# Moving two weight splits to GpSimd, dropping the pre-filled pad rows, and reordering the hand-over to the expert stage

## The chip, the core and the metric

The kernel runs on one core of a Trainium2 chip. The metric is the device time of one execution in microseconds (us). The engines are named as in the profile: PE is TensorE, DVE is VectorE, ACT is ScalarE, POOL is GpSimd, SP is SyncE, which here only issues DMAs. PEld is the weight load of TensorE, which overlaps with PE.

## The reference

Three stages run one after the other, all in fp32. The first is a linear attention with a decay for each head (batch 4, 8 heads, 768 positions, head size 64). The second is an MLP with a leaky ReLU whose slope is given for each feature (3072 tokens, 512 to 2048 to 512). The third is a mixture of 8 experts, in which each token goes to the one expert with the highest score.

```python
# attention, for each position t
state = gamma * state + outer(k[t], v[t]);  y[t] = scale * q[t] @ state
# MLP
h = x @ w_in;  g = maximum(h, 0) + alpha * minimum(h, 0);  x = g @ w_out
# experts
logits = normalise(x) @ normalise(expert_emb).T / tau
expert_idx = argmax(logits);  gate_w = softmax(logits)[expert_idx]
for e in range(8):
    mask = expert_idx == e
    out[mask] = gate_w[mask] * (maximum(x[mask] @ w1[e], 0) @ w2[e])
```

## The kernel before

**Products in parts.** A product in full precision is made of three matmuls of a high part (the value rounded to fp32r) and a low part (the value minus its high part): high by high, high by low, low by high. So each operand is split once. ACT makes the high part with a copy, and DVE or POOL makes the low part with a subtraction.

**Attention and MLP.** The 768 positions are 6 chunks of 128 (`NC = 6`), each with the 4 batches side by side, so that a chunk has 512 tokens. For each chunk come the attention (4 head pairs) and then the MLP, which this text calls an MLP pass. A pass has 16 blocks `f` of 128 hidden features. In block f, PE computes `hidden(f+1)` (12 matmuls, line 675) and `down(f)` (12 matmuls, line 684). DVE forms the leaky ReLU from the hidden product in lines 898 and 903, ACT makes its high part (line 1266) and POOL its low part (`g_lo`, line 1478; in blocks 0 and 15 DVE makes it, line 909). `down(f)` waits for the low part.

**The router in the next pass.** The scores of chunk c are computed during the MLP pass of chunk c + 1, on DVE, as products of 512 columns summed into one number (line 960): 4 in each of the blocks 1 to 7, 2 in the blocks 0 and 8, one in eight of them with an operand in PSUM. They follow the leaky ReLU of the same block in DVE's order. In blocks 9 to 12 DVE normalises, chooses the expert, and computes the table row of each token. POOL scatters the rows to their places in a table in DRAM (`scatter`, line 1496) with an indirect DMA. In the passes before the last one, POOL also scales queries and values for the next attention (lines 1461 and 1456) behind `g_lo` in blocks 3, 5, 6, 8 and 11.

**The table.** Each expert has a region of 3200 rows (`CAP`). Tokens are read from it in tiles of 128 rows, and the rest of an expert's last tile must hold pad rows. For this the kernel before writes 512 pad rows (`FILL`) at the start of each region, in the second chunk (line 506, 8 DMAs of 1028 KB), and once the counts are known 128 more behind the tokens of each expert (`pads`, line 380, 8 DMAs of 257 KB, each after a `value_load` of its address). So the tiles 2 and 3, which lie in the first 512 rows of the first expert, are loaded ahead of `pads` (`load_rows`, line 367), and tile 4 after it. The first expert, the one with most tokens, is chosen two chunks early (`choose_first`); its tiles 0 and 1 are loaded in the last MLP pass.

**The first expert's weights.** Four pieces `raw[0..3]` of 128x2048 are loaded and split in the last MLP pass: ACT makes the high parts in blocks 4, 5, 11 and 12 (`HI_AT`), and DVE the low parts in blocks 11 to 14 (`LO_VECTOR_AT`, `split_raw`, line 1026), counted in the semaphore `s_plV`.

**The expert stage.** For each tile t, PE computes `up(t, half)` twice (12 matmuls each, line 759), transposes the ReLU of it (`h_transpose(t)`, line 770), and computes `expert_down(t)` (24 matmuls, line 785). ACT and DVE each make one half of the ReLU (`relu_half`), and then the high (`h_hi_part`, line 1365) and the low part (`h_lo_part`, line 1130) of its transpose. `x_transpose(t)` (line 660) turns the token rows, and `x_hi_part` and `x_lo_part` split them. `y_part(t)` scales the result. The output bank is one, so `expert_down(t + 1)` waits for `y_part(t)`.

**The hand-over.** The order of each engine is written out by hand (lines 801 to 829 for PE, 1142 to 1203 for DVE, 1383 to 1402 for ACT, 515 to 541 for SP). PE does `up(0,0)`, transposes the rows of the last chunk and computes its logits with 32 matmuls of 8 columns (line 639), then `up(0,1)`, the rank and the counts (lines 646, 647 and 810), `up(1,0)`, `h_transpose(0)`, `up(1,1)`, and then the first down products. DVE turns the counts into the tile table: line 1160 writes the pad addresses (`s_pt`), and line 1195 the last entries (`s_tab`). Loads of token rows from tile 2 on wait for the table, and so does `up(2)`.

## Time and profile before

| | us |
|---|---|
| median of 3 executions | 992.1 |
| lowest, highest | 989.66, 993.94 |
| the profiled execution | 989.66 |
| its span, first to last instruction | 987.8 |
| PE busy in the span | 960.6 (97%) |
| DVE, ACT, POOL busy | 579.2, 256.5, 241.3 |
| share of PE in the chain that ended last | 88% |
| mean granted clock of TensorE, of full speed | 0.993 |

The profiled execution was also the fastest of the three. Its span leaves out 1.9 us around the instructions. An engine's busy time is the union of its instructions, so 97% says that PE has little idle time left, and not that its matmuls run at their peak. "Idle before" an instruction is told with its releaser, the instruction whose semaphore came last. A duration of POOL or DVE contains the time in which it was held back by the other one. The granted clock is 1.00 at 2.4 GHz and 0.50 at 1.2 GHz.

### The profile page before, as it was taken

How to read it: one execution, taken by the hardware profiler on the slowest of the kernel's cores; microseconds unless marked ns; L12 is line 12 of the kernel's file. 1: busy time of each engine (PE TensorE's matmuls, PEld its weight loads, DVE VectorE, ACT ScalarE, POOL GpSimd, SP SyncE). 2: the span in 40 equal slices, each digit the busy share in tenths (PEclk: the TensorE clock that was granted, in tenths of full speed). 3: DMA queues.
4: the chain of work that ended last, by engine and by line, in shares of the span. 5: the costliest groups of instructions: out<-in, count | busy, mean ns of one | idle time of the engine just before them, and what ended most of it. 6: DMA issues, size and time to landing. Idle time of an engine off the chain costs nothing.

```text
span 987.8 us, 16560 instructions
## 1 busy us (share of the span) xinstructions
PE 960.6 (97%) x5448; PEld 794.4 (80%) x5449; DVE 579.2 (59%) x1079; ACT 256.5 (26%) x405; POOL 241.3 (24%) x192
## 2 busy tenths in 40 slices
PE   7999999999999999999999999999999999999994
PEld 6788778888887888878887888877888888888883
DVE  4655579637973698459864878664332742524541
ACT  4222121112111211122111212332333533423541
POOL 3443114241433133413441224210000110000000
PEclk9999999999999999999999999999999999999998
DMA  7431393023001400140011203446331361423310
GB/s 283 157 139 55 116 370 114 1 86 129 0 0 73 140 0 0 43 149 1 1 44 54 107 35 134 130 136 249 128 128 43 150 262 43 175 75 121 125 44 31
DMA packets 27122, 100.48 MB, mean 102 GB/s; under 512 B 4383, under 2 KB 4767, under 8 KB 22448
## 3 DMA queue, kind: packets, MB, share of 16 engines
q1 hardware_dynamic: 19136, 80.64, 22.8%
q0 software_dynamic: 4336, 12.61, 3.3%
q10 hardware_dynamic: 3600, 6.58, 2.4%
q8 instruction: 29, 0.48, 0.2%
q14 instruction: 21, 0.17, 0.1%
HBM read 87.19 MB, written 24.20 MB: 113 GB/s over the span
## 4 chain that ended last, share of the span: by engine, by line
PE 88%; DVE 4%; DMA 2%; SPq 1%; ACT 1%; issue 1%; POOL 1%; ACTq 0%; DVEq 0%; POOLq 0%
PE bank L684 25%; PE bank L675 25%; PE bank L759 14%; PE bank L785 14%; PE bank L571 2%; PE bank L770 2%; PE bank L617 2%; PE bank L587 1%; PE bank L660 1%; PE bank L604 1%; DMA en_all<-en_rows 1%; DVE scratch L898 1%; DVE scratch L903 1%; DMA en_all<-in_qk 1%; DVE activations_split L909 1%
## 5 line engine op out<-in xcount | busy, mean ns | idle before, releaser
L684 PE MATMUL bank<-weights_split,activations_split 128*128 128x512 f32 x1152 | 278.7, 391 | 4.9 <-DVE activations_split L909 4.7
L675 PE MATMUL bank<-activations_split,weights_split 128*128 128x512 f32 x1152 | 277.5, 391 | 0.4 <-issue 0.4
L684 PEld LDWEIGHTS bank<-weights_split,activations_split 128*128 128x128 f32 x1152 | 215.2, 188 | 54.6 <-DVE activations_split L909 7.8
L675 PEld LDWEIGHTS bank<-activations_split,weights_split 128*128 128x128 f32 x1152 | 215.1, 188 | 45.8 <-issue 1.5
L1478 POOL TENSOR_TENSOR activations_split<-scratch,activations_split 128x512 fp32r<-128x512 f32 x84 | 118.0, 1405 | 332.5 <-ACT activations_split L1266 325.1
L1266 ACT CAST activations_split<-scratch 128x512 fp32r<-128x512 f32 x96 | 59.8, 622 | 418.1 <-DVE scratch L903 418.1
L785 PE MATMUL bank<-weights_split,activations_split 128*128 (+1 forms) x648 | 154.9, 394 | 3.0 <-DVE activations_split L1130 2.2
L759 PE MATMUL bank<-weights_split,activations_split 128*128 (+1 forms) x648 | 156.8, 398 | 0.5 <-DVE activations_split L1107 0.5
L785 PEld LDWEIGHTS bank<-weights_split,activations_split 128*128 128x128 f32 x648 | 119.6, 188 | 27.5 <-issue 3.6
L759 PEld LDWEIGHTS bank<-weights_split,activations_split 128*128 128x128 f32 x648 | 121.3, 191 | 24.8 <-issue 0.7
L960 DVE SCALAR_TENSOR_TENSOR attention<-rows,en_all 128x512 f32<-128x512 f32 x140 | 135.0, 1006 | 0.0
L898 DVE TENSOR_SCALAR scratch<-bank,alpha 128x512 f32<-128x512 f32 x96 | 71.8, 748 | 105.6 <-PE bank L675 101.6
L1532 POOL DMA_INDIRECT out<-scratch,y_token x27 | 29.1, 1079 | 297.9 <-ACT scratch L1375 297.9
L1130 DVE TENSOR_TENSOR activations_split<-bank,activations_split 128x512 fp32r<-128x512 f32 x54 | 34.8, 686 | 111.2 <-ACT activations_split L1365 111.1
L903 DVE SCALAR_TENSOR_TENSOR scratch<-bank,scratch 128x512 f32<-128x512 f32 x96 | 66.4, 692 | 3.3
L1121 DVE TENSOR_TENSOR weights_split<-attention,weights_split 128x2048 f32 (+1 forms) x21 | 47.6, 2288 | 15.5 <-ACT weights_split L1346 15.5
L1114 DVE TENSOR_SCALAR en_all<-bank 128x512 f32<-128x512 f32 x27 | 18.6, 690 | 50.2 <-PE bank L759 50.2
L863 DVE SCALAR_TENSOR_TENSOR attention<-bank,constants 128x512 f32<-128x512 f32 x44 | 28.4, 686 | 33.2 <-PE bank L571 33.2
L1375 ACT ACTIVATE scratch<-bank,rows 128x512 f32<-128x512 f32 x25 | 17.2, 687 | 93.8 <-PE bank L785 93.8
L1365 ACT CAST activations_split<-bank 128x512 fp32r<-128x512 f32 x54 | 29.0, 590 | 42.7 <-issue 29.6
L1346 ACT CAST weights_split<-attention 128x2048 f32 (+1 forms) x21 | 39.4, 1912 | 0.1
L1496 POOL DMA_INDIRECT expert_rows<-rows,slot_i x24 | 25.4, 1060 | 31.1 <-issue 28.3
(183 smaller groups left out, 678.4 us busy)
## 6 DMA issues: line engine op xcount, KB each, us to landing
attention<-in_w_exp SPq DMA_DIRECT2D x24, 1024.0 KB, 4.8
attention<-in_kv SPq DMA_DIRECT2D x43, 256.0 KB, 3.8
expert_rows<-in_pad_rows SPq DMA_DIRECT2D x8, 1028.0 KB, 18.3
en_all<-in_w_exp SPq DMA_DIRECT2D x8, 1024.0 KB, 7.1
rows<-in_w_mlp SPq DMA_DIRECT2D x14, 512.0 KB, 3.4
rows<-expert_rows ACTq DMA_DIRECT2D x25, 257.0 KB, 2.7
attention<-in_qk SPq DMA_DIRECT2D x12, 512.0 KB, 4.9
scratch<-in_qk SPq DMA_DIRECT2D x10, 512.0 KB, 3.7
```

Of the source, the lines that this page charges most:

```text
L675: last = mm(H_ps[f % 2][:, :], win(a, kc, f), x[:, kc, :], start=(k == 0), stop=(k == 3 * KC - 1))
L684: last = mm(bank[j][:, :], x[f % 2][:, j * P:(j + 1) * P], wout(a, f), start=(f == 0 and n == 0), stop=(f == FB - 1 and n == 2))
L759: last = mm(EH_ps[half][:, :], x[tt % 2][:, kc * P:(kc + 1) * P], W[:, bass.ds(slot * HALF + w1_at(kc, a) + half * 512, 512)], start=(k == ...
L785: last = mm(EY_ps[:, :], x[tt % 2][:, fc * P:(fc + 1) * P], W[:, bass.ds(slot * HALF + w2_at(fc, a), DM)], start=(k == 0), stop=(k == 3 * ...
L898: ve.tensor_scalar(neg, H_ps[f % 2][:, :], 0.0, alpha_sb[:, f:f + 1], ALU.min, ALU.mult)\
L903: ve.scalar_tensor_tensor(g_sb[f % 2], H_ps[f % 2][:, :], 0.0, neg, ALU.max, ALU.add)\
L960: ve.scalar_tensor_tensor(dot_out[n % 2], xrow[j][:, 0:DM], 1.0, EN[:, e * DM:(e + 1) * DM] if e < E - 1 else EN_ps, ALU.mult, ALU.mult, a ...
L1121: ve.tensor_tensor(W[:, bass.ds(at_ + CH, CH)], raw[m], W[:, bass.ds(at_, CH)].bitcast(f32), ALU.subtract).then_inc(s_lo[m // HC], 1)
L1130: ve.tensor_tensor(eh_lo[tt % 2][:, half * 512:(half + 1) * 512], HT_ps[half][:, :], eh_hi[tt % 2][:, half * 512:(half + 1) * 512].bitcast ...
L1266: se.copy(g_hi[f % 2], g_sb[f % 2]).then_inc(s_gh, 1)
L1346: se.copy(W[:, bass.ds((e % 2) * HALF + raw_at(m), CH)], raw[m]).then_inc(s_hi[m // HC], 1)
L1478: gp.tensor_tensor(g_lo[f % 2], g_sb[f % 2], g_hi[f % 2].bitcast(f32), ALU.subtract)\
```

## The change

- The 8 DMAs with 512 pad rows each are gone (`FILL`, `s_fill`, and the scatter's wait for it), and the pad array has 128 rows. `table_done` now also waits for `s_pads`; SP issues `pads` first, and then the rows of tiles 2, 3 and 4.
- The low parts of pieces 0 and 1 of the first expert are made on POOL in four halves of 128x1024, in blocks 5 to 8 of the last MLP pass, behind `g_lo`. DVE keeps pieces 2 and 3 in blocks 13 and 14.
- PE: `up(1,0)` comes ahead of the rank and the counts; `h_transpose(1)` comes behind `expert_down(0)` and no longer in the middle of it.
- DVE: `h_lo_part(0)` comes earlier in the table's chain, and `relu_half(1)` and the split of expert 1's piece 0 come behind its end, ahead of `h_lo_part(1)`.
- ACT: `y_part(0)` comes ahead of `h_hi_part(1)`, whose wait is now for `expert_down(0)`.

```diff
-    FILL = pad_rows.shape[0]
@@ table_done
         eng.wait_ge(s_tab, due(s_tab, 1))
+        eng.wait_ge(s_pads, due(s_pads, 16 * E))
@@
     HI_AT = {4: 0, 5: 1, 11: 2, 12: 3}
-    LO_VECTOR_AT = {11: 0, 12: 1, 13: 2, 14: 3}
+    LO_POOL_AT = {5: (0, 0), 6: (0, 1), 7: (1, 0), 8: (1, 1)}
+    LO_VECTOR_AT = {13: 2, 14: 3}
@@ sync
             chunk(1)
-            for e in range(E):
-                sp.dma_start(table[e * CAP:e * CAP + FILL, :], pad_rows[:, :]).then_inc(s_fill, 16)
             with sp.Fori(2, NC - 2) as c:
@@
                 sp.wait_ge(s_phi, due(s_phi, m + 1))
-                sp.wait_ge(s_plV, due(s_plV, m + 1))
+                if m < 2:
+                    sp.wait_ge(s_plP, due(s_plP, 2 * m + 2))
+                else:
+                    sp.wait_ge(s_plV, due(s_plV, m - 1))
                 load_raw(e, m)
-            table_done(sp)
-            load_rows(sp, 0, 2)
-            load_rows(sp, 0, 3)
             pads(sp)
             sp.wait_ge(s_pad0, due(s_pad0, 16))
-            sp.wait_ge(s_pads, due(s_pads, 16 * E))
-            load_rows(sp, 1, 0)
+            table_done(sp)
+            for t in range(2, 5):
+                load_rows(sp, t // 4, t % 4)
@@ tensor
             pe.wait_ge(s_phi, due(s_phi, 2))
-            pe.wait_ge(s_plV, due(s_plV, 2))
+            pe.wait_ge(s_plP, due(s_plP, 4))
             up(0, 0, 0, 0)
@@
             up(0, 0, 1, 0)
+            up(1, 1, 0, 0)
             router_rank(NC - 1)
             mm(CNT_ps, ones, seen[:, :, B], start=True, stop=True).then_inc(s_cnt, 1)
-            up(1, 1, 0, 0)
             h_transpose(0)
             up(1, 1, 1, 0)
             pe.wait_ge(s_phi, due(s_phi, NCH))
-            pe.wait_ge(s_plV, due(s_plV, NCH))
-            expert_down(0, 0, 0, between=lambda: h_transpose(1))
+            pe.wait_ge(s_plV, due(s_plV, 2))
+            expert_down(0, 0, 0)
+            h_transpose(1)
             expert_down(1, 1, 0, between=lambda: x_transpose(0, 2))
@@ vector
-            ve.scalar_tensor_tensor(tab[o, T_PADS:T_PADS + E], cnt[o, :], float(FILL), base[o, :], ALU.max, ALU.add).then_inc(s_pt, 1)
+            ve.tensor_tensor(tab[o, T_PADS:T_PADS + E], cnt[o, :], base[o, :], ALU.add).then_inc(s_pt, 1)
...
             link(ve.tensor_reduce(cnt_at[o, 0:1], eq_first[o, :], AX, ALU.add))
+            h_lo_part(0, 0)
...
             link(ve.tensor_copy(tab[o, T_EXP:T_EXP + TILES], eid[o, 1:TILES + 1]))
-            h_lo_part(0, 0)
...
             link(ve.tensor_scalar(tab[o, T_ROW:T_ROW + TILES], row_f[o, :], row_first[o, 0:1], float(PAD), ALU.add, ALU.min))
-            relu_half(1)
...
             ve.tensor_copy(tab[o, T_NEXT:T_NEXT + TILES], nx[o, :]).then_inc(s_tab, 1)
+            relu_half(1)
+            split_expert(1, (0,))
             h_lo_part(1, 1)
-            split_expert(1, (0,))
             x_lo_part(2, 2)
@@ scalar, h_hi_part and the order
-                    act.wait_ge(s_M2, due(s_M2, t - 1 if isinstance(t, int) and t == 1 else t))
+                    act.wait_ge(s_M2, due(s_M2, t))
...
             split_expert(1, (2, 3))
+            y_part(0, 0, 0)
             h_hi_part(1, 1)
-            y_part(0, 0, 0)
@@ gpsimd, mlp
+                    if is_last(c) and f in LO_POOL_AT:
+                        split_raw(*LO_POOL_AT[f])
@@
+            def split_raw(m, half):
+
+                pool.wait_ge(s_phi, due(s_phi, m + 1))
+                at_, n = raw_at(m) + half * CH // 2, CH // 2
+                gp.tensor_tensor(W[:, at_ + CH:at_ + CH + n], raw[m][:, half * n:(half + 1) * n],
+                                 W[:, at_:at_ + n].bitcast(f32), ALU.subtract).then_inc(s_plP, 1)
+
             def scatter(c, tiles=range(B)):
                 pool.wait_ge(s_rk, due(s_rk, c + 1))
-                pool.wait_ge(s_fill, due(s_fill, 16 * E))
@@ host
-    pad_rows = np.zeros((4 * P, DM + 2), np.float32)
+    pad_rows = np.zeros((P, DM + 2), np.float32)
```

## Rows read from the trace of the kernel before

**Rows 1.** Timeline, last MLP pass, blocks 5 and 6 (start us, length us, engine).

```profile
570.00 0.75 DVE L898 TENSOR_SCALAR scratch<-bank,alpha 128x512 f32<-128x512 f32 x1 [0.77 <-PE bank L675]
...
572.21 1.64 POOL L1478 TENSOR_TENSOR activations_split<-scratch,activations_split 128x512 fp32r<-128x512 f32 x1 [4.15 <-ACT activations_split L1266]
...
575.24 2.88 PE L684 MATMUL bank<-weights_split,activations_split 128*128 128x512 f32 x12
575.44 0.75 DVE L898 TENSOR_SCALAR scratch<-bank,alpha 128x512 f32<-128x512 f32 x1 [0.42 <-PE bank L675]
```

**Rows 2.** Timeline, the MLP pass before it, blocks 5 to 8.

```profile
466.59 0.75 DVE L898 TENSOR_SCALAR scratch<-bank,alpha 128x512 f32<-128x512 f32 x1 [0.21 <-PE bank L675]
...
472.35 0.74 DVE L898 TENSOR_SCALAR scratch<-bank,alpha 128x512 f32<-128x512 f32 x1
...
475.80 1.75 POOL L1461 TENSOR_TENSOR attention<-attention,constants 128x512 f32<-128x512 f32 x1
...
478.02 0.74 DVE L898 TENSOR_SCALAR scratch<-bank,alpha 128x512 f32<-128x512 f32 x1
...
485.14 1.30 POOL L1478 TENSOR_TENSOR activations_split<-scratch,activations_split 128x512 fp32r<-128x512 f32 x1 [3.30 <-ACT activations_split L1266]
...
486.39 1.05 POOL L1456 TENSOR_TENSOR attention<-attention,constants 128x512 f32<-128x512 f32 x1
```

**Rows 3.** All instructions of line 1510; duration in ns.

```profile
L1510 POOL TENSOR_TENSOR weights_split<-scratch,weights_split x1: 2360/2360/2360, 16.7 to 16.7; 128x1024 fp32r<-128x1024 f32 x1
```

**Rows 4.** Timeline, last MLP pass, blocks 11 to 14.

```profile
608.35 2.88 PE L684 MATMUL bank<-weights_split,activations_split 128*128 128x512 f32 x12
...
610.71 2.28 DVE L1026 TENSOR_TENSOR weights_split<-attention,weights_split 128x2048 fp32r<-128x2048 f32 x1
610.76 3.38 POOL L1478 TENSOR_TENSOR activations_split<-scratch,activations_split 128x512 fp32r<-128x512 f32 x1 [4.56 <-ACT activations_split L1266]
...
614.19 3.04 PE L684 MATMUL bank<-weights_split,activations_split 128*128 128x512 f32 x12 [0.24 <-POOL activations_split L1478]
...
625.47 2.88 PE L684 MATMUL bank<-weights_split,activations_split 128*128 128x512 f32 x12
```

**Rows 5.** Busy us of PE, PEld, DVE, ACT, POOL; granted clock, DMA share, GB/s.

```profile
640.00:646.00 6.00, 6.00 (x18) 4.84 (x17) 2.91 (x19) 1.09 (x2) 0.00 (x0) 0.50 0.00 0
```

**Rows 6.** Timeline of TensorE, from the last logits to the fourth up product.

```profile
640.13 5.47 PE L759 MATMUL bank<-weights_split,activations_split 128*128 128x512 f32 x12
...
652.83 2.89 PE L785 MATMUL bank<-weights_split,activations_split 128*128 128x512 f32 x12
...
660.18 2.99 PE L785 MATMUL bank<-weights_split,activations_split 128*128 128x512 f32 x12 [0.82 <-issue]
...
663.01 0.60 PE L660 MATMUL bank<-constants,rows 128*128 128x128 f32 x4
...
673.19 1.09 PE L770 MATMUL bank<-constants,en_all 128*128 128x128 f32 x8 [0.96 <-ACT en_all L1341]
...
674.78 5.72 PE L759 MATMUL bank<-weights_split,activations_split 128*128 x24 [0.49 <-DVE activations_split L1107]
```

**Rows 7.** Timeline of VectorE in that stretch.

```profile
647.28 0.15 DVE L1160 SCALAR_TENSOR_TENSOR tile_table<-cnt,constants 1x8 int32<-1x8 f32 x1
...
654.95 0.17 DVE L1195 CAST tile_table<-nx 1x31 int32<-1x31 f32 x1
```

**Rows 8.** Timeline of SyncE's DMA issues in that stretch.

```profile
655.92 1.42 SPq L367 DMA_DIRECT2D rows<-expert_rows  x2
658.12 10.16 SPq L380 DMA_DIRECT2D expert_rows<-in_pad_rows  x8
```

**Rows 9.** The chain that ended last, one piece (start us, length us, what).

```profile
667.75 3.71 DMA expert_rows<-in_pad_rows
```

**Rows 10.** DMA issues by line: count, size, median us to landing.

```profile
rows<-expert_rows SPq DMA_DIRECT2D x3, 257.0 KB, 2.6
```

**Rows 11.** Timeline of TensorE, second MLP pass, first down product.

```profile
134.68 3.01 PE L684 MATMUL bank<-weights_split,activations_split 128*128 128x512 f32 x12 [1.97 <-DVE activations_split L909]
```

More of the change, by code:

```diff
@@ L293, in build @@
     s_emb_ld, s_en_st, s_en_all, s_en_last = sem("emb_ld"), sem("en_st"), sem("en_all"), sem("en_last")
-    s_star, s_tail, s_fill = sem("star"), sem("tail"), sem("fill")
+    s_star, s_tail = sem("star"), sem("tail")
     s_lg = sem("lg")
@@ L311, in build @@
     s_raw = [sem(f"raw{i}") for i in range(4)]
-    s_phi, s_plV = sem("phi"), sem("plV")
+    s_phi, s_plV, s_plP = (sem(n) for n in ("phi", "plV", "plP"))
     s_hi, s_lo = ([sem(f"{part_}_{w}") for w in ("w1", "w2")] for part_ in ("hi", "lo"))
@@ L379, in pads @@
             r = eng.value_load(tab[0:1, T_PADS + e:T_PADS + e + 1], min_val=0, max_val=PAD - P)
-            eng.dma_start(table[bass.ds(r, P), :], pad_rows[0:P, :]).then_inc(s_pads, 16)
+            eng.dma_start(table[bass.ds(r, P), :], pad_rows[:, :]).then_inc(s_pads, 16)
     def is_last(c):
@@ L483, in spread_en @@
                   .then_inc(s_en_all, 16)
-                sp.dma_start(table[PAD:PAD + P, :], pad_rows[0:P, :]).then_inc(s_pad0, 16)
+                sp.dma_start(table[PAD:PAD + P, :], pad_rows[:, :]).then_inc(s_pad0, 16)
             def chunk(c, following=True, with_k=True):
```

## The prediction, made before the changed kernel ran

> **What bounds the kernel now.** I read the page first: PE is busy for 97% of the span and carries 88% of the chain that ended last. So an edit pays or costs only by the idle or slow time of PE that it removes or adds. PE's waits by releaser come next, and they are short everywhere. Then I read the timeline at the three places that the change touches: the last MLP pass, the hand-over to the experts, and the second pass, where the 512-row fills are issued. The reader is to see three things. In the last pass PE runs at a fixed pace of 5.44 us for a block (the distance of two L898 in [rows 1]). `g_lo` of block 5 is ready at 573.85 and its down product starts at 575.24, so POOL and DVE have a slack of 1.39 us. In [rows 4] a DVE split and a POOL subtraction that start together take 2.28 and 3.38 us, while the POOL one alone takes 1.30 [rows 2]: one of the two engines is held until the other is done, if both of the DVE instruction's operands lie in SBUF.
>
> **Part A, low parts on POOL in blocks 5 to 8.** A half of 128x1024 took 2.36 us on POOL [rows 3], in the stage where nothing stood beside it. Four are added, each behind `g_lo`, and DVE's score products of the block stand beside them: two SBUF operands each, but for one in eight. The pass before shows what one POOL instruction at that place does: with a decay of 1.05 us behind `g_lo` in block 5, DVE's block took 472.35 - 466.59 = 5.76 us, and in block 6 with one of 1.75 us, 478.02 - 472.35 = 5.67 us [rows 2]. The 1.75 contains a wait of 0.45 for DVE (1.30 alone), and I give the 1.05 and the 2.36 the same wait: 1.50 and 2.81. So a block of DVE becomes 5.76 + 2.81 - 1.50 = 7.07 us in blocks 5 and 7, and 5.67 + 2.81 - 1.75 = 6.73 us in block 6, where PE wants 5.44. DVE starts the blocks 6, 7 and 8 late by 1.63, 2.92 and 4.55 us. The slack is 1.39 us in block 7 and 0.34 more in blocks 6 and 8, in which the second product reads PSUM and doesn't delay `g_lo` (its 1.64 in [rows 1] against 1.30 in [rows 2]). So PE waits 0 us in block 6, 2.92 - 1.39 = 1.53 in block 7, and 4.55 - 1.73 - 1.53 = 1.29 in block 8. After a short wait PE loses some more, for its weight load wasn't ahead: the block of [rows 4] has a wait of 0.24 and is 614.19 - 608.35 = 5.84 us, 0.40 over the pace. I add 0.16 twice or nothing, 2.8 to 3.1, and take +3.0. In block 9 the fourth half still holds POOL, but only small DVE chains follow, and a block of slack with them. Bounds: 0, if all four fit in, and +4.6, if DVE's whole lag of block 8 reached PE.
>
> **Part B, DVE free in blocks 11 and 12.** From the down product of block 11 to that of block 14 it is 625.47 - 608.35 = 17.12 us, and three blocks at the pace are 16.32 [rows 4]. The 0.80 begins with the split at 610.71, which holds `g_lo` of block 12, and with it the two scatters behind it on POOL. That split goes; the one of block 13 stays, but it starts behind 1.4 us of ReLU and holds `g_lo` only until some 5.0 us into the block, 0.2 under the deadline. I take -0.8 (bounds -0.8 and 0).
>
> **Part C, the hand-over.** `up(1,0)` moves ahead of the rank, which waited for nothing there. Before it, PE runs at half clock: the granted clock is 0.50 from 640 to 646 [rows 5], 12 matmuls take 5.47 us at 640.13, and the same count 2.89 later [rows 6]. PE itself gains about 0.2, since the small matmuls of the rank leave the slow stretch. But rank and counts come about 2.8 us later, which is a full product less that gain, and so does all that DVE derives from them.
>
> First its order. The pad addresses are there at 647.43 + 2.8 = 650.2 [rows 7]. `h_lo_part(0)`, two instructions of 512 columns (0.7 us each, as L898 in [rows 1]), now starts at about 651.1, since it moves up; the first down product at 652.7 (652.83 before) finds it ready, and 24 matmuls, twice the 2.7 of [rows 6], end at 658.2. The table's end moves from 655.12 to about 657.4. Then DVE does `relu_half(1)` (0.7), the split (2.28, the size of L1026 in [rows 4]), and `h_lo_part(1)`, whose first half is ready at about 661.0. `h_transpose(1)` ends at 659.2, so PE waits 1.8 us for a low part that lay beside the down product before. Before, the second down product started at 660.18 after a wait of 0.82 for `y_part(0)` [rows 6]. Now it starts at 661.0: +0.8.
>
> Then the loads. SP moves `pads` ahead of the rows. The rows' first load was issued 655.92 - 655.12 = 0.80 after the table [rows 7, 8], which is the cost of a `value_load`. Eight pads took 10.16 us, issue by issue [rows 8], and the last landed 3.71 us after 667.75 [rows 9]. After: first issue 651.0, last 660.7, landed 664.4. Row issue 665.2, and the rows land 2.6 us later [rows 10], at 667.8. PE wants to transpose tile 2 in the middle of the second down product, which was at 663.01, 2.83 us behind its start [rows 6], and is now at 663.8. It waits 4.0 us. Queued behind that transpose on PE are the second half of `expert_down(1)` and all the tiles; nothing else can fill in.
>
> One stall goes. Before, ACT waited for `s_pads` ahead of `relu_half(2)`, and the transpose of tile 3 and the fourth up product were late by it (PE waits of 0.96 at 673.19 and 0.49 at 674.78 [rows 6]). Now the pads are done by then, but the ReLU and the x parts still follow up(2) directly, so that of these 1.45 I count 1.3 as gained. Sum of C at the fourth up product (674.78 before): +0.8 + 4.0 - 1.3 = +3.5. Bounds: -0.6, if the rows come in time, and +5, if pads beside the scatters take 1.5 us longer.
>
> **Part D, no fills.** Nothing but the next chunk's loads stands behind them on SP. The broadcast of the expert embeddings was issued before them and was still under way; PE waited 1.97 us for what hangs on it [rows 11]. If fills took bandwidth from it, up to 1.97 less the 0.2 or so of an ordinary restart comes back, 1.7; the first issued is likely served first, so I take 0. The scatter's wait for them was long fulfilled.
>
> **Sum.** +3.0 - 0.8 + 3.5 = +5.7 us. On the profiled execution that is 989.66 + 5.7 = 995.4. This one was the fastest of three, 2.4 us under the median of 992.1, so for a median I predict 992.1 + 5.7 = 997.8.
>
> **The rivals.** (1) *The rows of tile 2 come in time.* Place: the transpose in `expert_down(1)`. It decides at 663.8 minus 2.6, 661.2: if SP issues the rows by then, the 4.0 of C goes, and with it the loss of 1.45 before; C is -0.6 and the sum 3.0 - 0.8 - 0.6 = +1.6, 993.7, no slower than a measurement can tell. It needs pads at some 0.8 us each instead of 1.38 ((10.16 - 0.5)/7). For it speaks that the pads no longer share SP with row loads in front of them; against it that the `value_load` of 0.80 and the issue itself stay. (2) *The lock costs PE nothing.* A is 0, by DVE or POOL taking turns otherwise: -0.8 + 3.5 = +2.7, 994.8. Against it stand the 5.76 and 5.67, already over 5.44 with half the work. (3) *The clock falls in the new wait.* PE idles for 4 us in the middle of a product, with 1.8 us of idle 3 us before. The nearest rows: 1.97 us of idle [rows 11] behind which 12 matmuls took the usual 3.0 us, and 0.50 behind the tiny logit matmuls [rows 5]. A product of 12 took 2.6 more then, so +8.3, 1000.4, and two such products 1003. The Trainium skill, "TensorE: Matmul & The Clock Gate", section "Why this matters for your kernels", asks to keep idle gaps between bursts of matmuls short, or the clock goes back to half; by that rule rival 3 is the outcome. No row here has such a gap. (4) *Fills held the broadcast*: -1.7 on the forecast, 996.1.
>
> **How the numbers follow.** Chances: forecast 0.38 (995.8 to 999.8), rival 1 0.20, rival 2 0.12, rival 3 0.20, rival 4 0.05, and 0.05 for something that gains, as the slow stretch at 640 not coming back (3 us) on top of rival 1. A measurement of this kernel tells 0.5%, 5 us, from no change, so slower begins at 997.1. The forecast lies 0.7 above this: 0.25 of its 0.38 is slower, and with rival 3 and a remainder of 0.01 it is 0.46. Faster is 0.05, and the rest, 0.49, is the same. The range of 991.5 to 1002 leaves out half of the gains, some of rival 1's lower side, and the two-product case of rival 3.
>
> **What would show it.** Right: waits of PE at L684 for POOL L1478 in blocks 7 and 8 of the last pass, some 1.5 and 1.3 us; DVE blocks of about 7 us there; no wait in blocks 12 to 14; a wait of about 1.8 us ahead of the second down product, and one of about 4 us at L660 for the DMA of tile 2's rows; pads issued from 651 on. Wrong: A falls if blocks 5 to 8 keep 5.44 us each. C falls if the row DMA is issued before 661, or if PE's wait for it is under 1 us. The size is wrong if the granted clock is below 1 anywhere between 655 and 680, or if PE's wait at 134.68 has changed.

## The result and the profile after

The changed kernel takes 999.32 us in the median (996.05 to 1003.19, 7 runs), and the one before 990.33 (988.94 to 993.94, 7 runs). The ratio is 1.0088, with a 95% interval of 1.0061 to 1.0114: slower by 0.9%. The profiled execution took 999.35 us, its span is 997.4, so it stands at the median, while the one of before (989.66) is 0.7 us under its own. Between the two profiles lie 9.6 us of span, and 9.0 us between the medians.

The first line of the changed kernel's page, busy time of each engine, share of the span and instructions:

```profile
PE 963.7 (97%) x5448; PEld 796.2 (80%) x5449; DVE 582.8 (58%) x1077; ACT 256.6 (26%) x405; POOL 249.1 (25%) x196
```

PE's busy share still reads 97%. Both stages that the change touches must be read in the timeline. First the blocks 5 to 9 of the last MLP pass, which answer to [rows 1] and [rows 2]. L899 is the old L898, L961 the old L960, L1479 the old L1478, and L1498 the new split on POOL.

```profile
570.03 0.75 DVE L899 TENSOR_SCALAR scratch<-bank,alpha 128x512 f32<-128x512 f32 x1 [0.76 <-PE bank L675]
...
573.83 2.84 POOL L1498 TENSOR_TENSOR weights_split<-attention,weights_split 128x1024 fp32r<-128x1024 f32 x1
574.36 2.87 DVE L961 SCALAR_TENSOR_TENSOR attention<-rows,en_all 128x512 f32<-128x512 f32 x1
...
575.27 2.88 PE L684 MATMUL bank<-weights_split,activations_split 128*128 128x512 f32 x12
...
577.16 0.74 DVE L899 TENSOR_SCALAR scratch<-bank,alpha 128x512 f32<-128x512 f32 x1
...
583.94 0.74 DVE L899 TENSOR_SCALAR scratch<-bank,alpha 128x512 f32<-128x512 f32 x1
...
587.79 3.01 PE L684 MATMUL bank<-weights_split,activations_split 128*128 128x512 f32 x12 [1.34 <-POOL activations_split L1479]
...
591.02 0.74 DVE L899 TENSOR_SCALAR scratch<-bank,alpha 128x512 f32<-128x512 f32 x1
...
594.54 3.01 PE L684 MATMUL bank<-weights_split,activations_split 128*128 128x512 f32 x12 [1.02 <-POOL activations_split L1479]
...
600.12 2.88 PE L684 MATMUL bank<-weights_split,activations_split 128*128 128x512 f32 x12
```

DVE's blocks take 7.13, 6.78 and 7.08 us now (570.03 to 577.16, 583.94 and 591.02), and PE waits 1.34 and 1.02 us for `g_lo` in blocks 7 and 8. The score product that starts at 574.36, while POOL's split runs, takes 2.87 us where the same product takes 0.68 us with POOL idle. From the down product of block 5 to that of block 9 it is 24.85 us, where the pace of 5.44 us for a block gives 21.76. Then blocks 11 to 14, which answer to [rows 4]:

```profile
611.46 2.88 PE L684 MATMUL bank<-weights_split,activations_split 128*128 128x512 f32 x12
...
627.78 2.88 PE L684 MATMUL bank<-weights_split,activations_split 128*128 128x512 f32 x12
```

That is 16.32 us, exactly three blocks at the pace, with no wait left. The hand-over on PE answers to [rows 6]:

```profile
642.09 7.36 PE L759 MATMUL bank<-weights_split,activations_split 128*128 128x512 f32 x24
...
653.52 5.61 PE L785 MATMUL bank<-weights_split,activations_split 128*128 128x512 f32 x24
...
661.62 3.01 PE L785 MATMUL bank<-weights_split,activations_split 128*128 128x512 f32 x12 [1.63 <-DVE activations_split L1131]
670.36 1.08 PE L660 MATMUL bank<-constants,rows 128*128 128x128 f32 x4 [5.73 <-issue]
671.09 4.03 PE L785 MATMUL bank<-weights_split,activations_split 128*128 128x512 f32 x12
...
682.77 5.72 PE L759 MATMUL bank<-weights_split,activations_split 128*128 x24 [0.75 <-DVE activations_split L1108]
```

The second down product waits 1.63 us for DVE, and the transpose of tile 2 waits 5.73 us (the profile puts it down to "issue" and names no engine; the rows that it needs were issued by SP at 667.60, see below). SP in the same stretch, to compare with [rows 8]:

```profile
651.73 12.69 SPq L380 DMA_DIRECT2D expert_rows<-in_pad_rows  x8
667.60 2.58 SPq L366 DMA_DIRECT2D rows<-expert_rows  x3
```

The first pad is issued at 651.73, but all 8 take 12.69 us, and the rows of tiles 2, 3 and 4 follow from 667.60; PE starts on tile 2 at 670.36, 2.76 us later. VectorE, which answers to [rows 7]:

```profile
650.82 0.15 DVE L1161 TENSOR_TENSOR tile_table<-cnt,constants 1x8 int32<-1x8 f32 x1
...
657.90 0.17 DVE L1195 CAST tile_table<-nx 1x31 int32<-1x31 f32 x1
...
660.79 1.28 DVE L1131 TENSOR_TENSOR activations_split<-bank,activations_split 128x512 fp32r<-128x512 f32 x2
```

`h_lo_part(1)` at 660.79 starts 2.89 us behind the table's last entry at 657.90; a ReLU and a weight split stand between them. The pad addresses are written at 650.82. The table is complete at 658.07, 9.5 us ahead of the load of tile 2's rows, so that load did not wait for the table but for the pads: SP stood 2.2 us at their semaphore after it had issued the last of them. The granted clock in four stretches (busy time of PE, PEld, DVE, ACT, POOL, then the clock, the DMA share, GB/s), and the last down product, first of the changed kernel and then of the one before:

```profile
642.00:646.00 4.00, 4.00 (x13) 3.16 (x13) 2.62 (x18) 1.31 (x2) 0.00 (x0) 0.57 0.00 0
664.00:670.00 6.00, 0.63 (x3) 0.19 (x1) 0.00 (x0) 0.00 (x0) 0.00 (x0) 0.99 0.49 162
670.00:673.00 3.00, 2.64 (x9) 2.29 (x10) 0.90 (x2) 0.68 (x2) 0.00 (x0) 0.50 0.90 216
980.00:983.00 3.00, 3.00 (x10) 2.33 (x9) 0.69 (x1) 0.00 (x0) 0.00 (x0) 0.58 0.08 27
```

```profile
979.55 7.35 PE L785 MATMUL bank<-weights_split,activations_split 128*128 x24 [2.17 <-DVE activations_split L1131]
971.56 5.74 PE L785 MATMUL bank<-weights_split,activations_split 128*128 x24 [2.17 <-DVE activations_split L1130]
```

In the first of them the slow stretch of the logits is there again, but shorter than in [rows 5]. In the second PE idles, and the clock falls at its end. In the third the second half of the down product runs at 0.50. The last product takes 7.35 us for 24 matmuls: the clock was still 1.00 when it started and fell right behind that. The kernel before has the same wait of 2.17 us ahead of this product, and there the clock stayed at 1.00 (5.74 us).

The 9.6 us by stretch, each from the starts in the two traces:

| stretch of PE | before | after | difference |
|---|---|---|---|
| up to the down product of block 5, last pass | 575.24 | 575.27 | 0.0 |
| block 5 to block 9 | 21.76 | 24.85 | +3.1 |
| block 11 to block 14 | 17.12 | 16.32 | -0.8 |
| `up(0,0)` to the first down product | 21.02 | 19.39 | -1.6 |
| first to second down product | 7.35 | 8.10 | +0.75 |
| second down product to the transpose of tile 2 | 2.83 | 8.74 | +5.9 |
| that transpose to `up(2)` | 3.18 | 4.60 | +1.4 |
| `up(2)` to `up(3)` | 8.59 | 7.81 | -0.8 |
| the last down product | 5.74 | 7.35 | +1.6 |

The first row hides two that cancel: the changed kernel was 1.57 us ahead at the first down product of the second pass (133.11 against 134.68 in [rows 11]), and lost that right behind it to a clock that fell there. The product (from the chain that ended last) and the clock in that stretch:

```profile
133.11 4.60 PE bank L684 x12
```

```profile
134.00:138.00 4.00, 4.00 (x12) 3.11 (x11) 3.96 (x9) 1.25 (x3) 1.60 (x1) 0.58 0.00 0
```

The kernel before takes 3.01 us for the same 12 matmuls.

### The profile page after: what moved, and what is told of

Same layout as the page of the kernel before. It is cut to its first block, busy times and chain, and to the rows that moved or that the text cites. A ratio compares the mean times of both kernels' runs of the same rounds, so it can differ in the third digit from the quotient of the medians.

```text
span 997.4 us, 16552 instructions
## 1 busy us (share of the span) xinstructions
PE 963.7 (97%) x5448; PEld 796.2 (80%) x5449; DVE 582.8 (58%) x1077; ACT 256.6 (26%) x405; POOL 249.1 (25%) x196
## 4 chain that ended last, share of the span: by engine, by line
PE 88%; DVE 4%; issue 2%; DMA 2%; POOL 2%; ACT 1%; SPq 0%; ACTq 0%; DVEq 0%; POOLq 0%
PE bank L684 24%; PE bank L675 23%; PE bank L759 15%; PE bank L785 15%; PE bank L571 2%; PE bank L770 2%; PE bank L617 2%; PE bank L587 1%; PE bank L660 1%; PE bank L604 1%; DMA en_all<-en_rows 1%; DVE scratch L899 1%; POOL weights_split L1498 1%; DVE scratch L904 1%; DVE activations_split L910 1%
## 5 line engine op out<-in xcount | busy, mean ns | idle before, releaser
L1479 POOL TENSOR_TENSOR activations_split<-scratch,activations_split 128x512 fp32r<-128x512 f32 x84 | 117.3, 1396 | 327.4 <-ACT activations_split L1267 315.2
L961 DVE SCALAR_TENSOR_TENSOR attention<-rows,en_all 128x512 f32<-128x512 f32 x140 | 141.6, 1053 | 0.0
L899 DVE TENSOR_SCALAR scratch<-bank,alpha 128x512 f32<-128x512 f32 x96 | 71.8, 748 | 105.8 <-PE bank L675 102.0
L1366 ACT CAST activations_split<-bank 128x512 fp32r<-128x512 f32 x54 | 29.0, 590 | 39.1 <-issue 27.3
L1336 ACT CAST activations_split<-bank 128x512 fp32r<-128x512 f32 x29 | 16.9, 586 | 61.5 <-PE bank L660 61.5
```

What stands on the lines that cost most here:

```text
L899: ve.tensor_scalar(neg, H_ps[f % 2][:, :], 0.0, alpha_sb[:, f:f + 1], ALU.min, ALU.mult)\
L961: ve.scalar_tensor_tensor(dot_out[n % 2], xrow[j][:, 0:DM], 1.0, EN[:, e * DM:(e + 1) * DM] if e < E - 1 else EN_ps, ALU.mult, ALU.mult, a ...
L1479: gp.tensor_tensor(g_lo[f % 2], g_sb[f % 2], g_hi[f % 2].bitcast(f32), ALU.subtract)\
```

## The experiments

All are compared with the kernel before on the same chip; the ratio is that of the times, with its 95% interval. The line numbers of a kernel shift with its edits. Where two experiments differ by 3.5 us or less, their intervals mostly touch or overlap, and the trace carries the argument more than the time does.

**split_only.** Of the change only the splits on POOL.

```diff
-    LO_VECTOR_AT = {11: 0, 12: 1, 13: 2, 14: 3}
+    LO_POOL_AT = {5: (0, 0), 6: (0, 1), 7: (1, 0), 8: (1, 1)}
+    LO_VECTOR_AT = {13: 2, 14: 3}
```

> The kernel before with the split of pieces 0 and 1 moved to POOL in blocks 5 to 8 of the last MLP pass, and nothing else. Theory (the lock between POOL and DVE makes DVE's blocks 7 us long): PE waits for g_lo in blocks 7 and 8, some 1.3 and 1.0 us, the stretch from the down product of block 5 to that of block 9 is 24.8 us instead of 21.8, the 0.8 us of blocks 12 to 14 go, and the kernel is about 2.3 us slower than before. Rival (the lock is absorbed, and all of the loss is made in the hand-over): 0.8 us faster, with 21.8 us from block 5 to block 9.

Measured: 992.28 us, ratio 1.0029 (1.0014 to 1.0045), 2.9 us slower. The down products in its timeline:

```profile
573.79 2.88 PE L688 MATMUL bank<-weights_split,activations_split 128*128 128x512 f32 x12
...
586.30 3.02 PE L688 MATMUL bank<-weights_split,activations_split 128*128 128x512 f32 x12 [1.35 <-POOL activations_split L1482]
...
593.06 3.02 PE L688 MATMUL bank<-weights_split,activations_split 128*128 128x512 f32 x12 [1.01 <-POOL activations_split L1482]
...
598.64 2.88 PE L688 MATMUL bank<-weights_split,activations_split 128*128 128x512 f32 x12
```

From block 5 to block 9 it is again 24.85 us, with the two waits of the changed kernel. So the loss of 3.1 us in this stretch belongs to this edit alone.

**handover_only.** The changed kernel with the splits of before.

```diff
-    LO_POOL_AT = {5: (0, 0), 6: (0, 1), 7: (1, 0), 8: (1, 1)}
-    LO_VECTOR_AT = {13: 2, 14: 3}
+    LO_VECTOR_AT = {11: 0, 12: 1, 13: 2, 14: 3}
```

> The changed kernel with the splits of pieces 0 and 1 back on DVE in blocks 11 and 12; the fills are gone, and the hand-over is the changed one. Theory (the rows of tile 2 come late): PE waits 4 to 6 us at the transpose of tile 2 and 1.6 to 1.8 us ahead of the second down product, and the kernel is 5 to 7 us slower than before, and about 2.3 faster than the changed one. Rival (both parts lean on each other, as a later pass makes a later table): the sum of this and the one with the splits alone is not the whole.

Measured: 995.14 us, ratio 1.0053 (1.0031 to 1.0076), 5.2 us slower. The second down product, the transpose of tile 2 and the second half of the product:

```profile
659.26 3.01 PE L781 MATMUL bank<-weights_split,activations_split 128*128 128x512 f32 x12 [1.62 <-DVE activations_split L1127]
667.19 1.08 PE L656 MATMUL bank<-constants,rows 128*128 128x128 f32 x4 [4.92 <-issue]
667.92 4.70 PE L781 MATMUL bank<-weights_split,activations_split 128*128 128x512 f32 x12
```

A wait of 1.62 and one of 4.92 us, and then 12 matmuls in 4.70 us, at half clock for most of them. With split_only it makes 2.9 + 5.2 = 8.1 of the 8.7 us: the two parts add up within their intervals.

**split_late.** The changed kernel, POOL's halves three blocks later.

```diff
-    LO_POOL_AT = {5: (0, 0), 6: (0, 1), 7: (1, 0), 8: (1, 1)}
+    LO_POOL_AT = {8: (0, 0), 9: (0, 1), 10: (1, 0), 11: (1, 1)}
```

> The changed kernel with POOL's four halves in blocks 8 to 11 instead of 5 to 8, where DVE has no score products but only 2 in block 8. Theory (the lock against the products is the cost, and not POOL's time): no wait of PE for POOL in blocks 6 to 11, about 3 us faster than the changed kernel. Rival (POOL's own 2.4 us behind g_lo is too much for a block): waits of PE for POOL in blocks 9 to 12, and no gain.

Measured: 995.62 us, ratio 1.0059 (1.0041 to 1.0077), against 1.0088 (1.0061 to 1.0114) of the changed kernel. That would be 2.9 us of its loss gone, but the intervals overlap, so the trace has to show it.

```profile
593.10 2.88 PE L684 MATMUL bank<-weights_split,activations_split 128*128 128x512 f32 x12
...
604.44 3.06 PE L684 MATMUL bank<-weights_split,activations_split 128*128 128x512 f32 x12 [0.30 <-POOL activations_split L1479]
```

The down products of blocks 8 and 10: no wait in the one, 0.30 us in the other, instead of 1.34 and 1.02. From block 5 to block 11 PE loses 0.6 us against its pace, and in the changed kernel 3.1. POOL does the same four halves behind `g_lo`. So it isn't POOL's time that costs most, but DVE's products that it holds back, as the theory says. That PE would not wait for POOL at all was missed by this 0.30.

**order_only.** The kernel before with the changed order on PE, DVE and ACT; the fills and SP's order stay. PE's part of the edit:

```diff
+            up(1, 1, 0, 0)
             router_rank(NC - 1)
             mm(CNT_ps, ones, seen[:, :, B], start=True, stop=True).then_inc(s_cnt, 1)
-            up(1, 1, 0, 0)
...
-            expert_down(0, 0, 0, between=lambda: h_transpose(1))
+            expert_down(0, 0, 0)
+            h_transpose(1)
```

> The kernel before with the changed order on PE, DVE and ACT in the hand-over, while the fills, SP's order and the splits stay. Theory (the order costs 0.8 us at the second down product and the loads the rest): a wait of 1.6 to 1.8 us ahead of the second down product, no wait of more than 0.5 at the transpose of tile 2, since its row is loaded ahead of the pads, and 0 to 2 us slower than before. ACT now waits for pads that start even later than before, so the wait of 1.0 us at the third transpose of the ReLU should grow by up to 2.5. Rival (the order itself is what costs): 5 us or more over before, with the clock falling again.

Measured: 991.61 us, ratio 1.0018 (1.0003 to 1.0032), 1.8 us slower.

```profile
649.68 5.61 PE L785 MATMUL bank<-weights_split,activations_split 128*128 128x512 f32 x24
...
657.79 3.01 PE L785 MATMUL bank<-weights_split,activations_split 128*128 128x512 f32 x12 [1.62 <-DVE activations_split L1131]
660.64 0.60 PE L660 MATMUL bank<-constants,rows 128*128 128x128 f32 x4
...
672.71 1.97 PE L770 MATMUL bank<-constants,en_all 128*128 128x128 f32 x8 [2.85 <-ACT en_all L1342]
```

The second down product comes 8.11 us behind the first, after a wait of 1.62. Tile 2's transpose doesn't wait. The third transpose of the ReLU waits 2.85 us instead of 0.96 [rows 6], since ACT stands at `s_pads`, and the pads start as late as before (657.63 against 658.12 [rows 8]). The clock fell behind that wait (0.58 from 672 to 674).

**loads_only.** The kernel before without the fills and with SP's new order; PE, DVE and ACT as before.

```diff
-                sp.dma_start(table[e * CAP:e * CAP + FILL, :], pad_rows[:, :]).then_inc(s_fill, 16)
...
-            table_done(sp)
-            load_rows(sp, 0, 2)
-            load_rows(sp, 0, 3)
             pads(sp)
             sp.wait_ge(s_pad0, due(s_pad0, 16))
-            sp.wait_ge(s_pads, due(s_pads, 16 * E))
-            load_rows(sp, 1, 0)
+            table_done(sp)
+            for t in range(2, 5):
+                load_rows(sp, t // 4, t % 4)
```

> The kernel before without the fills and with SP's new order (pads first, then the rows of tiles 2, 3 and 4), while PE, DVE, ACT and the splits are those of before. Theory (the pads stand ahead of the rows, and a part of the row's wait is theirs alone): the pads start near 648 and end near 659, the rows land near 665, PE waits 2 to 3.5 us at the transpose of tile 2, ACT's wait for the pads at the third transpose goes (1.5 us), and the kernel is 1 to 2.5 us slower than before; the first down product of the second pass waits its 1.8 to 2.0 us as before, since the fills held nothing. Rival (only the late counts make the rows late): no wait over 0.5 us at the transpose of tile 2, and 1 us or more faster than before.

Measured: 993.15 us, ratio 1.0031 (1.0011 to 1.0050), 3.1 us slower, more than the 1 to 2.5 expected.

```profile
661.09 3.00 PE L781 MATMUL bank<-weights_split,activations_split 128*128 128x512 f32 x12 [0.82 <-issue]
666.86 0.63 PE L656 MATMUL bank<-constants,rows 128*128 128x128 f32 x4 [2.77 <-issue]
667.24 4.58 PE L781 MATMUL bank<-weights_split,activations_split 128*128 128x512 f32 x12
```

```profile
649.29 11.03 SPq L380 DMA_DIRECT2D expert_rows<-in_pad_rows  x8
```

The wait is 2.77 us, inside the expected, and the half clock in the 12 matmuls behind it (4.58 us instead of 3.0) is what the expectation had left out. PE's wait at the product behind the broadcast is 2.06 us here, 1.97 in [rows 11] and 1.83 in the changed kernel. Over all traces it is 1.40 to 2.63 us in the eight kernels with the fills and 1.29 to 2.40 in the five without, and the product starts at 133.19 to 134.82 us with them and at 133.01 to 134.49 without. An effect of the fills is not seen in this spread, and one of a few tenths is not excluded; the 1.57 us by which the changed kernel was ahead there lie in it.

order_only and loads_only make 1.8 + 3.1 = 4.9 of the 5.2 us of handover_only. That their times add up is in part chance, for the waits do not: tile 2's transpose waits 0 us in the one and 2.77 in the other, and 4.92 with both edits together. Late counts cost nothing at tile 2 as long as its rows go ahead of the pads; behind the pads they cost another 2.2 us.

**rank_first.** The changed kernel with the rank and the counts ahead of `up(1,0)` again.

```diff
             up(0, 0, 1, 0)
-            up(1, 1, 0, 0)
             router_rank(NC - 1)
             mm(CNT_ps, ones, seen[:, :, B], start=True, stop=True).then_inc(s_cnt, 1)
+            up(1, 1, 0, 0)
```

> The changed kernel with the rank and the counts back ahead of up(1,0) on PE; all else is the changed one. Theory (the late counts make the pads, and the pads make the rows of tile 2 late): the first pad is issued about 2.8 us earlier against the end of the logits, PE's wait at the transpose of tile 2 falls from 5 to 6 us to 2 to 3, and the kernel is 2 to 3 us faster than the changed one. Rival (the wait is set by the table or by the transfers themselves): the wait stays over 4.5 us.

Measured: 994.63 us, ratio 1.0053 (1.0039 to 1.0068), a loss some 3.4 us smaller than the changed kernel's, with intervals that overlap a little.

```profile
667.39 0.78 PE L660 MATMUL bank<-constants,rows 128*128 128x128 f32 x4 [2.58 <-issue]
```

Tile 2's transpose waits 2.58 us instead of 5.73. Not all of these 3.15 us are the order's. The first pad is issued at 649.75 and not at 651.73, 2.0 us earlier; the eight pads take 11.10 us and not 12.69, 1.6 less; and the gap from their end to the first row load is 0.6 longer. Against the end of the logits the first pad came only 1.6 us earlier, where 2.8 was expected, mostly since all of `up(0,1)` ran at half clock here (5.47 us).

**best1.** The kernel before with other means for the two gains that the trace offers.

```diff
-    LO_VECTOR_AT = {11: 0, 12: 1, 13: 2, 14: 3}
+    LO_VECTOR_AT = {8: 0, 11: 1, 13: 2, 14: 3}
...
-            act.wait_ge(s_pads, due(s_pads, 16 * E))
             w1_part(next_expert(2), 1)
             relu_half(2)
             x_hi_part(3, 3)
+            act.wait_ge(s_pads, due(s_pads, 16 * E))
```

> The kernel before with two edits and none of the change: DVE splits piece 0 in block 8, where it has only two score products, and piece 1 in block 11, and ACT waits for the pads behind relu_half(2) and the high part of tile 3, ahead of its first row load. Theory (what the change was after can be had without the lock and without late rows): blocks 12 to 14 lose their 0.8 us, the waits of 1.0 and 0.5 us at the third transpose and the fourth up product fall to 0 and about 0.5, 2.1 us faster than before. Rival (a split on DVE in block 8 holds g_lo or the ReLU of block 9): a wait of PE in block 8 or 9, and 1 us or less gained.

Measured: 986.76 us, ratio 0.9970 (0.9956 to 0.9985).

```profile
588.79 3.04 DVE L1026 TENSOR_TENSOR weights_split<-attention,weights_split 128x2048 fp32r<-128x2048 f32 x1
...
591.42 2.88 PE L684 MATMUL bank<-weights_split,activations_split 128*128 128x512 f32 x12
```

```profile
671.52 5.73 PE L759 MATMUL bank<-weights_split,activations_split 128*128 x24 [0.78 <-DVE activations_split L1107]
```

DVE's split in block 8 waits for `g_lo` (3.04 us instead of 2.28), and the next down product isn't late. The blocks 11 to 14 lose nothing any more, 0.8 us gained. The fourth up product waits 0.78 us for the low part of tile 3, and comes 7.83 us behind the third instead of 8.59, a gain of 0.8 where 1.3 was expected. By the ratio the kernel is some 3 us faster; the trace shows 1.6 of them as gained by the edits, which the interval (1.5 to 4.4 us) allows, and another 1.6 in a slow stretch at the logits that was shorter in this execution.

**best1_again.** The same kernel a second time.

> The kernel best1 once more, beside best3 on the same chip. Theory: 0.2 to 0.4% faster than before again. Rival: the 0.3% of the first time were the state of the clock in those executions, and the ratio is 0.999 or more.

Measured: 985.84 us, ratio 0.9972 (0.9956 to 0.9988). The gain is there a second time, on another chip, and the ratio of 0.999 or more that the rival asks for lies outside both intervals.

**interleave.** The kernel before with up products among the logits.

```diff
-            for j in range(B):
-                last_logits(j)
+            last_logits(0)
+            last_logits(1)
             up(0, 0, 1, 0)
+            last_logits(2)
+            last_logits(3)
+            up(1, 1, 0, 0)
             router_rank(NC - 1)
             mm(CNT_ps, ones, seen[:, :, B], start=True, stop=True).then_inc(s_cnt, 1)
-            up(1, 1, 0, 0)
```

> The kernel before with up(0,1) between the second and the third of the four logit products, and up(1,0) behind the fourth, ahead of the rank. Theory (the clock falls because 32 matmuls of 8 columns follow each other for 4 us, at a point of the clock's own time that differs from run to run): no granted clock under 1 between 635 and 650, up to 3 us faster where the run before had the slow stretch and nothing where it had none, 1 to 2 us in the median; the counts come no later than before. Rival (the fall comes from something else in this stage, or the ranks now come late): the slow stretch stays, or a wait of over 1 us at the rank or behind it.

Measured: 993.28 us, ratio 1.0042 (1.0027 to 1.0056): slower, a miss.

```profile
637.36 3.04 PE L759 MATMUL bank<-weights_split,activations_split 128*128 128x512 f32 x12
...
651.30 4.58 PE L785 MATMUL bank<-weights_split,activations_split 128*128 128x512 f32 x12 [1.95 <-DVE activations_split L1132]
...
675.71 7.31 PE L759 MATMUL bank<-weights_split,activations_split 128*128 x24 [0.46 <-DVE activations_split L1109]
```

The slow stretch at the logits is gone: `up(0,1)` took 3.04 us. But PE arrives early at the first down product and waits 1.95 us for `h_lo_part(0)`, which stands behind the table's experts in DVE's order, and the clock falls there (12 matmuls in 4.58 us) and again at the fourth up product (24 in 7.31). In this trace the time was not saved but moved. The two falls cost 1.7 and 1.6 us, which is more than the 2.5 us by which this profile's span is longer; why the median is 4 us slower is left open.

**best2.** Both edits of best1 with this order.

> The kernel before with both edits of best1 and the order of interleave. Theory (they don't touch each other): the sum of the two, 3 to 4 us faster than before. Rival: the later ranks use up the time that the late wait for the pads has given, and the sum is under 2 us.

Measured: 988.78 us, ratio 0.9994 (0.9983 to 1.0005). It has the same wait of 1.95 us at the first down product, with 12 matmuls in 4.58 us behind it, and the sum that the theory expected didn't come.

**best3.** best2, with DVE's order mended.

```diff
             link(ve.tensor_reduce(cnt_at[o, 0:1], eq_first[o, :], AX, ALU.add))
+            h_lo_part(0, 0)
...
             link(ve.tensor_copy(tab[o, T_EXP:T_EXP + TILES], eid[o, 1:TILES + 1]))
-            h_lo_part(0, 0)
+            relu_half(1)
...
-            relu_half(1)
```

> The kernel best2 with h_lo_part(0) right behind the counts of the first expert, as the changed kernel has it, and relu_half(1) behind the table's experts. Theory (the order of interleave lost its gain at the first down product, which waited 1.95 us for this low part): no wait over 0.3 us at the first down product, the fourth up product 1.5 to 2 us earlier than in best2, 4 to 5 us faster than before. Rival (the clock falls somewhere else in the hand-over whenever the logits come in two parts): the waits are gone but half clock shows up in it, and it is no faster than best1.

Measured: 985.20 us, ratio 0.9955 (0.9939 to 0.9971), the lowest of all; the changed kernel's is 1.0088.

```profile
647.69 2.88 PE L785 MATMUL bank<-weights_split,activations_split 128*128 128x512 f32 x12
...
668.94 5.76 PE L759 MATMUL bank<-weights_split,activations_split 128*128 x24 [0.75 <-DVE activations_split L1109]
```

```profile
635.00:650.00 15.00, 15.00 (x86) 12.90 (x87) 9.15 (x47) 9.25 (x9) 3.01 (x4) 1.00 0.10 35
650.00:665.00 15.00, 14.18 (x69) 11.41 (x68) 9.07 (x16) 3.86 (x8) 3.29 (x3) 1.00 0.61 185
```

No wait ahead of the first down product, and the clock is at full in the whole hand-over. From `up(0,0)` to `up(3)` it is 39.3 us (629.68 to 668.94) against 43.0 before and 48.6 in the changed kernel. In best2 it is 43.0, so the fourth up product comes 3.7 us earlier, more than the 1.5 to 2 expected: the fall of the clock went with the wait. Beside best1 on the same chip it is ahead by 0.6 us in the median, and the intervals of their ratios overlap: the step from best1 to best3 is not shown to be a gain.

## Why the prediction was right

The direction, the range and the places were right, and the predicted 997.8 us lies 1.5 under the median. That it lies so near is in part luck: the difference was put at 5.7 us and is 9.0 between the medians, and the median of before turned out 1.8 us lower than the 992.1 from which the prediction started. What happened is the forecast's mechanism with rival 3 on top, and the sign that the prediction had named for a wrong size, a granted clock below 1 between 655 and 680, was met. By step:

- **Part A, the lock between POOL and DVE.** Predicted blocks of 7.07 and 6.73 us, waits of 1.53 and 1.29, and +3.0. Measured 7.13 and 6.78, 1.34 and 1.02, and +3.1, in the changed kernel and in split_only alone. The blocks of the pass before, with one shorter POOL instruction each, were enough to work out DVE's blocks. The +3.0 agrees better than its terms: the two waits make 2.36 us and not 2.82, and the matmuls around them lose 0.73 us (three down products of 3.01 us instead of 2.88, and later starts behind them), where the prediction had 0.3 or nothing. The two misses cancel. Rival 2 is out by the waits themselves; split_late shows that they come from DVE's products.
- **Part B.** Predicted -0.8, measured -0.80.
- **Part C, the order.** Predicted +0.8 at the second down product with a wait of 1.8, measured +0.75 with 1.63. The pad addresses came 2.8 us later in the prediction and 3.5 later in the traces (650.82 against 647.28 [rows 7]): 2.8 for the product that now stands ahead and 2.3 for the later start of the hand-over, less 1.6 for the shorter slow stretch of the logits. Against `up(0,0)` they are 1.2 later.
- **Part C, the loads.** This is the term that was mis-sized. Predicted 4.0 us of wait at tile 2, measured 5.9 more from the second down product to the transpose. I had taken the 10.16 us of eight pads from [rows 8]; in the changed kernel they took 12.69, with 2.98 us from the third issue to the fourth where the others lie 1.3 to 1.9 apart, and in the four other kernels that issue them at this point 11.0 to 11.2. The waits go with it: 4.9 us at 11.1 and 11.2 (handover_only, split_late), 5.7 at 12.7. What makes the hole was not tried; it stands in one execution's trace, so it can be a chance of that execution. The parts of the wait are the pads ahead of the rows (2.6 to 2.8 us, rank_first and loads_only), the late counts (another 2.2, handover_only against loads_only), and the hole (0.8).
- **The stall given back.** Predicted -1.3, measured -0.8: the fourth up product still waits 0.75 for tile 3.
- **Rival 3, the clock.** The forecast had no fall in the new wait and gave one a chance of 0.20. It came, in each of the traces with a long wait there: 1.4 us behind the wait of 5.7, 1.6 to 2.1 in handover_only, split_late, rank_first and loads_only, less than the 2.6 that I had set (each is the time from tile 2's transpose to `up(2)` less the 3.18 of before). The rule of the Trainium skill, "TensorE: Matmul & The Clock Gate", section "Why this matters for your kernels", to keep idle gaps between bursts of matmuls short, agrees with these traces; I should have given it more than a fifth.
- **Rivals 1 and 4** are out: no row of tile 2 came in time, and the product behind the broadcast waits 1.83 us, where rival 4 asked for 1.7 less than 1.97.
- **What no step had.** -1.6 us between `up(0,0)` and the first down product and +1.6 at the last product are the clock's. The first stretch takes 17.78 us at full clock with the changed order (order_only, split_late), 19.39 in the changed kernel and 20.94 in handover_only, which has the same instructions there. The two cancel here.

The sum was +5.7, and the spans differ by 9.6. The 3.9 that were missing are the loads (1.9), the clock at tile 2 (1.4), the smaller give-back (0.5), part A (0.1) and the two last, which cancel. For each term the prediction had only the one profiled execution of before.

## What to carry over

Work that is moved to an idle engine must be priced with what it holds: GpSimd was idle for about 4 us of each block (3.8 and 4.15 us ahead of `g_lo` in blocks 6 and 5), but with two SBUF operands on both sides it and VectorE took turns (a product of 0.68 us took 2.87), and VectorE was the one with a deadline. When a bulk write early in the kernel is dropped because a late one covers it, look at who stands behind the late one: no trace shows the 8 MB of fills to have cost anything beyond the spread, and the small writes that took their place stood ahead of the one load that TensorE needs next. And put a wait as far down an engine's order as the data allows: ACT's wait for the pads gave 0.8 us by moving behind three other lines.

## What was not expected of the hardware

- TensorE's clock went to 0.50 behind short waits, and not always behind the same one. At the first down product of the second pass it fell behind 1.83 us of idle in the changed kernel (0.58 in the mean of 134 to 138), 2.01 in best1_again, 2.06 in loads_only and 2.40 in split_late, and stayed at 1.00 behind 1.97 in the kernel before, 2.46 in interleave and 2.63 in order_only. Ahead of the last down product PE waits 2.16 or 2.17 us in all 13 traces; the 24 matmuls behind it took 7.3 to 7.4 us in seven of them and 5.7 to 5.8 in the other six. The 5.7, 4.9 and 2.6 to 2.8 us of idle at tile 2 were all followed by a fall.
- A fall cost 1.4 to 3.2 us in these traces. The spread of 5 to 7 us between the runs of the kernel before goes with the clock: of 29 executions of the kernel before on one chip, the five slowest (992.7 to 993.6 us) have a mean granted clock of 0.989 or 0.990, and the five fastest (986.8 to 987.4) 0.994 or 0.995.
- It also fell while PE was never idle, at 32 matmuls of 8 columns in a row (4 us), in the kernel before and in most others, but not in order_only and split_late, which run the same instructions there. With 12 full matmuls between two rows of 16 it stayed at 1.00 in interleave, best2 and best3.
- A subtraction of 1024 columns on POOL took 2.36 us alone and 2.84 behind a DVE product, and each DVE product with two SBUF operands that met it 2.87 instead of 0.68. A DVE product with one operand in PSUM took 0.68 beside POOL's subtraction.
